# First network of a two-network kernel: weight loads placed around a block's transfers, one semaphore per piece, and an earlier table read

## The reference, cut to what matters

```
# first network (a mixture of experts), N=3072, D=384, E=8, F=1024
expert_idx = argmax(normalised x @ normalised emb.T / tau)
for e in range(E):
    mask = expert_idx == e
    h = np.maximum(x[mask] @ w1[e], 0.0)
    out[mask] = gate_w[mask, None] * (h @ w2[e])
# second network, d_ff = 2048
h = x @ w_in
g = np.maximum(0.01 * h, h)
return g @ w_out
```

## Time and profile before

| What | Value |
|---|---|
| Median of 3 runs | 834.14 us (833.15 to 834.78) |
| Profiled execution, its own time | 836.12 us |
| Its span in the trace | 834.1 us |
| PE busy | 808.0 us, 97% of the span |
| DVE, ACT, POOL busy | 452.2, 345.8, 210.7 us |
| Mean granted TensorE clock | 0.992 |
| First network, about | 132.6 to 427.9 us of the span |

### The profile page before, as it was taken

The page is one execution under the profiler, slowest core; times in us unless marked ns, Lnnn a source line. Parts: engine busy times, 40 slices in busy tenths (PEclk is TensorE's granted clock), DMA queues, the critical chain, the costliest instruction groups (busy, mean ns, idle before and its releaser), DMA issues.

```text
span 834.1 us, 17016 instructions
## 1 busy us (share of the span) xinstructions
PE 808.0 (97%) x5259; PEld 721.7 (87%) x5260; DVE 452.2 (54%) x705; ACT 345.8 (41%) x643; POOL 210.7 (25%) x278
## 2 busy tenths in 40 slices
PE   7999999989989999899999999999999999999998
PEld 6888887978879989788889998998998998998997
DVE  7999986776467474574465433433533433443332
ACT  3555564555346354353254333323323333333223
POOL 5666623233234242332124003003003001000100
PEclk9999999999999999899999999999999999999999
DMA  9997663676787767887733201201101001000001
GB/s 224 261 265 238 202 218 131 219 265 202 285 289 245 245 224 232 283 235 257 222 91 41 39 1 39 39 1 38 28 10 38 0 0 38 1 1 8 30 1 39
DMA packets 64128, 108.97 MB, mean 131 GB/s; under 512 B 24199, under 2 KB 45747, under 8 KB 64080
## 3 DMA queue, kind: packets, MB, share of 16 engines
q1 hardware_dynamic: 54896, 93.47, 37.0%
q0 software_dynamic: 5888, 14.85, 5.6%
q10 hardware_dynamic: 3296, 0.06, 0.2%
HBM read 78.89 MB, written 30.85 MB: 132 GB/s over the span
## 4 chain that ended last, share of the span: by engine, by line
PE 64%; DMA 21%; SPq 6%; issue 4%; DVE 4%; POOL 1%; ACT 1%; DVEq 0%; POOLq 0%; ACTq 0%
PE bank L1747 24%; PE bank L1699 24%; DMA hidden_rows<-hs 18%; PE bank L1494 3%; PE bank L1534 3%; PE bank L1511 2%; PE bank L1672 2%; SPq L448 2%; PE bank L1652 2%; SPq L410 2%; PE bank L1500 1%; PE bank L1542 1%; DMA hds<-hidden_rows 1%; SPq L555 1%; PE bank L1554 1%
## 5 line engine op out<-in xcount | busy, mean ns | idle before, releaser
L1699 PE MATMUL bank<-yT,wts 128*128 128x512 f32 x864 | 217.1, 395 | 0.0
L1747 PE MATMUL bank<-wts,gs 128*128 128x384 f32 x1152 | 215.3, 335 | 0.4 <-ACT os L1010 0.2
L1747 PEld LDWEIGHTS bank<-wts,gs 128*128 128x128 f32 x1152 | 202.1, 188 | 10.7 <-issue 1.6
L1699 PEld LDWEIGHTS bank<-yT,wts 128*128 128x128 f32 x864 | 160.8, 188 | 30.6
L1289 DVE TENSOR_TENSOR g<-bank,small 128x512 f32<-128x512 f32 x96 | 66.4, 692 | 173.6 <-ACT small L919 173.5
L1652 PE MATMUL bank<-wts,gxT 128*128 (+1 forms) x549 | 137.8, 405 | 4.7 <-issue 4.7
L919 ACT ACTIVATE small<-bank 128x512 f32<-128x512 f32 x96 | 57.6, 599 | 184.7 <-PE bank L1699 184.2
L1652 PEld LDWEIGHTS bank<-wts,gxT 128*128 128x128 f32 x549 | 103.8, 194 | 28.1 <-issue 7.0
L1461 DVE TENSOR_TENSOR gs<-g,gs 128x512 fp32r<-128x512 f32 x96 | 66.6, 693 | 66.3 <-ACT gs L1021 66.3
L770 POOL DMA_INDIRECT out<-os,tokens x20 | 19.7, 986 | 285.5 <-ACT os L1010 280.9
L1021 ACT ACTIVATE gs<-g 128x512 fp32r<-128x512 f32 x96 | 60.7, 632 | 74.0 <-DVE g L1289 72.9
(11 more groups left out here) (179 smaller groups left out, 764.7 us busy)
## 6 DMA issues: line engine op xcount, KB each, us to landing
raw<-weights SPq DMA_DIRECT2D x60, 512.0 KB, 6.3
hidden_rows<-hs SPq DMA_DIRECT2D x29, 512.0 KB, 4.9
hds<-hidden_rows SPq DMA_DIRECT2D x29, 512.0 KB, 4.1
qkas<-qka SPq DMA_DIRECT2D x20, 675.5 KB, 5.9
vs<-v SPq DMA_DIRECT2D x24, 192.0 KB, 4.7
x_rows<-xs SPq DMA_DIRECT2D x24, 192.0 KB, 3.7
yl<-y_rows SPq DMA_DIRECT2D x20, 192.0 KB, 4.7
qkas<-qka SPq DMA_DIRECT2D x4, 227.5 KB, 6.8
```

Source lines behind the costliest of these rows:

```text
L1699: m = pe.matmul(gps[f % 2][:, :], wts[:, 0, w_part, n:n + P], yT[:, 1 - u, y_part, k], start=(k == 0 and (w_part, y_part) == (0, 0)), stop ...
L1747: m = pe.matmul(ops[tt], gs[:, f % 4, g_part, tt * P:(tt + 1) * P], wts[:, 1, w_part, f * D:(f + 1) * D], start=(f == 0 and (g_part, w_par ...
```

## The change

Weight loads: `load_half` becomes three calls of `load_piece`, and every piece has a semaphore of its own (`raw_in[0..5]`, count 16 per expert instead of 48 per half). A piece's load waits only for the rounding of the same piece of the expert before (`w_lo[half] >= n*3 - 2 + j`).

SP order: `load_next(m)` with all its loads becomes `load_next(m, j)` with one piece j of each half. It is called three times for a window: in front of the store (j=0), between the issue of the store and the wait for it (j=1), and behind the issue of the read (j=2). Each call reads the table again. The W2 load that was unconditional at window 5 is now at window 4. The four `load_quarter(1, j)` move from behind windows 27 to 30 to behind the loop.

Rounding order: on ACT and DVE the first two pieces of W1 are rounded ahead of `h_round`/`h_rest` of window w+1; the third W1 piece and W2 follow as before. In step 1 `h_round(2)`/`h_rest(2)` and `copy_ys` now come before the rounding of W2 instead of after.

PE: the expert numbers (table reads) of the step's hidden blocks and of window w are read at the start of the step, ahead of the waits for turned rows and weights.

```
         def split_hi(act, n, par, pieces):
             for j in pieces:
-                if j % 3 == 0:
-                    act.wait_ge(raw_in[j // 3], n * 48 + 48)
+                act.wait_ge(raw_in[j], n * 16 + 16)
...
+        def load_piece(eng, half, n, j):
+            eng.wait_ge(w_lo[half], n * 3 - 2 + j)
+            src = weights[n, half] if isinstance(n, int) else weights[ds(n, 1), half].rearrange("a p n -> (a p) n")
+            at = half * 3 + j
+            eng.dma_start(raw[:, at * PC:(at + 1) * PC], src[:, j * PC:(j + 1) * PC]).then_inc(raw_in[at], 16)
...
-            def load_next(m):
+            def load_next(m, j):
...
                 code = table(sp, m - 4)
                 last_first, fourth_first = sp.snap(code & (8 * E)), sp.snap(code & E)
                 with sp.If(last_first > 0):
-                    load_half(sp, 0, sp.snap((table(sp, m - 1) & (E - 1)) + 2))
+                    load_piece(sp, 0, sp.snap((table(sp, m - 1) & (E - 1)) + 2), j)
                 if isinstance(m, int) and m == FIRST + 2:
-                    return
-                if isinstance(m, int) and m == FIRST + 3:
-                    load_half(sp, 1, sp.snap((code & (E - 1)) + 2))
-                else:
+                    load_piece(sp, 1, sp.snap((table(sp, 1) & (E - 1)) + 2), j)
+                elif not (isinstance(m, int) and m == FIRST + 3):
                     with sp.If(fourth_first > 0):
-                        load_half(sp, 1, sp.snap((code & (E - 1)) + 2))
+                        load_piece(sp, 1, sp.snap((code & (E - 1)) + 2), j)
...
+            def move(w, u):
+                load_next(w, 0)
                 sp.wait_ge(h_turned, w * 2 - 2 * FIRST + 2)
...
                 sp.dma_start(h_rows[u], hs[:, u]).then_inc(h_stored[u], 16)
+                load_next(w, 1)
                 sp.wait_ge(h_stored[u], passed(w, u))
...
                 sp.dma_start(hds[:, u].rearrange("p (i n) -> p i n", i=QUADS), h_quarters[u]).then_inc(h_moved[u], 16)
+                load_next(w, 2)
...
-                elif w >= WINDOWS - QUADS:
-                    load_quarter(1, w - WINDOWS + QUADS)
+            wait_rows(1)
+            for j in range(QUADS):
+                load_quarter(1, j)
...
# ACT, and DVE alike with split_lo and h_rest
+                if ahead(w, 3) and not (isinstance(w, int) and w < CLOSE):
+                    with act.If(first3 > 0):
+                        first_weights(w + 3, act.snap(e + first1 // (2 * E) + first2 // (4 * E) + 2), W1_PIECES[:2])
+                if ahead(w, 1) and not (isinstance(w, int) and w == 0):
                     for half in range(2):
                         h_round(w + 1, 1 - u, half)
...
-                        first_weights(w + 3, act.snap(e + first1 // (2 * E) + first2 // (4 * E) + 2))
+                        first_weights(w + 3, act.snap(e + first1 // (2 * E) + first2 // (4 * E) + 2), W1_PIECES[2:])
...
# PE
             def step(w, u):
+                blocks = [(block, of(w, u, block), expert_of(block)) for block in hidden_blocks(w)]
+                e = expert_of(w)
```

More of the change, by code:

```diff
@@ L255, in build @@
         state_ready = sem("state_ready")
-        raw_in = [sem("raw_in0"), sem("raw_in1")]
+        raw_in = [sem(f"raw_in{j}") for j in range(PIECES)]
         w_hi = [sem("w1_hi"), sem("w2_hi")]
@@ L441, in split_lo @@
                                   ALU.subtract).then_inc(w_lo[j // 3], 1)
+        def load_piece(eng, half, n, j):
[3 more added lines that the diff above has]
+            eng.dma_start(raw[:, at * PC:(at + 1) * PC], src[:, j * PC:(j + 1) * PC]).then_inc(raw_in[at], 16)
         def load_half(eng, half, n):
-            eng.wait_ge(w_lo[half], n * 3)
-            src = weights[n, half] if isinstance(n, int) else weights[ds(n, 1), half].rearrange("a p n -> (a p) n")
             for j in range(3):
-                eng.dma_start(raw[:, (half * 3 + j) * PC:(half * 3 + j + 1) * PC],
-                              src[:, j * PC:(j + 1) * PC]).then_inc(raw_in[half], 16)
+                load_piece(eng, half, n, j)
         W1_PIECES, W2_PIECES = range(0, 3), range(3, 6)
@@ L513, in load_first @@
                 sp.dma_start(raw[:, c * PC:(c + 1) * PC],
-                             weights[0, half, :, part * PC:(part + 1) * PC]).then_inc(raw_in[half], 16)
+                             weights[0, half, :, part * PC:(part + 1) * PC]).then_inc(raw_in[c], 16)
             def step(c, b):
@@ L543, in _ @@
                 load_half(sp, half, 1)
-            def move_h(w, u):
+            def load_next(m, j):
+                if isinstance(m, int) and m == FIRST:
+                    with sp.If(sp.snap(table(sp, 0) & (2 * E)) > 0):
+                        load_piece(sp, 0, 3, j)
+                    return
+                if isinstance(m, int) and m == FIRST + 1:
+                    with sp.If(sp.snap(table(sp, 0) & (4 * E)) > 0):
+                        load_piece(sp, 0, sp.snap((table(sp, m - 1) & (E - 1)) + 2), j)
+                    with sp.If(sp.snap(table(sp, 0) & (2 * E)) > 0):
+                        load_piece(sp, 1, 2, j)
+                    return
+                code = table(sp, m - 4)
+                last_first, fourth_first = sp.snap(code & (8 * E)), sp.snap(code & E)
+                with sp.If(last_first > 0):
+                    load_piece(sp, 0, sp.snap((table(sp, m - 1) & (E - 1)) + 2), j)
+                if isinstance(m, int) and m == FIRST + 2:
+                    load_piece(sp, 1, sp.snap((table(sp, 1) & (E - 1)) + 2), j)
+                elif not (isinstance(m, int) and m == FIRST + 3):
+                    with sp.If(fourth_first > 0):
+                        load_piece(sp, 1, sp.snap((code & (E - 1)) + 2), j)
+            def move(w, u):
+                load_next(w, 0)
                 sp.wait_ge(h_turned, w * 2 - 2 * FIRST + 2)
@@ L613, in _ @@
                 move(w, w % 2)
-                if w in (20, WINDOWS - QUADS):
-                    wait_rows(w // (WINDOWS - QUADS))
+                if w == 20:
+                    wait_rows(0)
                 if w < 20 + QUADS:
                     load_quarter(0, w - 20)
-                elif w >= WINDOWS - QUADS:
-                    load_quarter(1, w - WINDOWS + QUADS)
+            wait_rows(1)
+            for j in range(QUADS):
+                load_quarter(1, j)
             for j in range(2):
@@ L894, in h_round, with first_weights @@
                 act.activation(by_square(ht_of(w, u)[:, 0, cols]), moved(u, half), ACT.Copy).then_inc(ht_hi, 1)
-            def first_weights(s, e):
+            def first_weights(s, e, pieces=W1_PIECES):
                 wait_from(act, h_ready, s * 2)
-                split_hi(act, e, next_set(act, e), W1_PIECES)
+                split_hi(act, e, next_set(act, e), pieces)
             def second_weights(w, e):
@@ L960, in step @@
                     scale_small(0)
-                if ahead(w, 1) and not (isinstance(w, int) and w < FIRST):
+                if ahead(w, 3) and not (isinstance(w, int) and w < CLOSE):
+                    with act.If(first3 > 0):
+                        first_weights(w + 3, act.snap(e + first1 // (2 * E) + first2 // (4 * E) + 2), W1_PIECES[:2])
+                if ahead(w, 1) and not (isinstance(w, int) and w == 0):
                     for half in range(2):
@@ L982, in step @@
                         second_weights(w, act.snap(e + 1))
-                if isinstance(w, int) and w == 1:
-                    for half in range(2):
-                        h_round(w + 1, 1 - u, half)
                 if not ahead(w, 1):
@@ L1422, in step @@
                     leaky(0)
-                if ahead(w, 1) and not (isinstance(w, int) and w < FIRST):
+                if ahead(w, 3) and not (isinstance(w, int) and w < CLOSE):
+                    with dve.If(first3 > 0):
+                        e2 = dve.snap(e + first1 // (2 * E) + first2 // (4 * E) + 2)
+                        split_lo(dve, e2, next_set(dve, e2), W1_PIECES[:2])
+                if ahead(w, 1) and not (isinstance(w, int) and w == 0):
                     for half in range(2):
                         h_rest(w + 1, 1 - u, half)
-                if not (isinstance(w, int) and w < FIRST):
+                if not (isinstance(w, int) and w == 0):
                     copy_ys(w, u)
@@ L1441, in step @@
                         split_lo(dve, e1, next_set(dve, e1), W2_PIECES)
-                if isinstance(w, int) and w < FIRST:
+                if isinstance(w, int) and w == 0:
                     copy_ys(w, u)
-                if isinstance(w, int) and w == 1:
-                    for half in range(2):
-                        h_rest(w + 1, 1 - u, half)
                 if isinstance(w, int) and w == WINDOWS - 2:
@@ L1701, in inner, with expert_of, block_hidden @@
                 m.then_inc(g_ready, 1)
-            def block_hidden(s, u, between=None):
-                e = pe.snap(table(pe, s) & (E - 1))
+            def expert_of(w):
```

(8 more changed lines are left out.)

22 lines of the change are left out of this document (2 added, 20 removed).

## The result

The changed kernel takes 828.25 us (median of 6 runs, 827.35 to 830.51) against 834.77 us for the kernel before: ratio 0.9921, 95% interval 0.9897 to 0.9945. It is faster by 6.5 us. The profiled execution took 827.88 us, its span is 826.1 us. The forecast was 825.

The account below looks back on a forecast made before the run. The prediction took SP's serial loop of stores, waits, reads and loads to pace the first network; its terms, 30.3 - 3.0 - 2.0 - 33.5 - 6 + 4 + 1.3 = -8.9 us, gave 825 us, 8-in-10 range 817 to 838.

Parts of the forecast that it names:

- The bound: First network: SP's serial loop of store, wait, read, table and loads sets the pace, 9.4 us a window against PE's 8.6.
- A: SP's loop: the added table-reading call behind the read is on the path in all 25 windows, +30.3 us.
- B: SP's load issues: one in three now lies under the store, W1's second table read is paid twice; -3.0 us.
- C: Quarter loads: three that stood in front of the stores of windows 28, 29, 30 leave the loop; -2.0 us.
- D: SP's stores with fewer loads in front, six becoming two and three becoming one, window 5 included: -33.5 us.
- E: Next store behind a read: later issue queues less, -6 us; third pieces standing in between cost +4 us.
- the third rival: SP's queue: same bytes, what one store gains the next loses, terms cancel, 834 us; chance 0.11.
- F: Start, step 1: W2 rounded behind h_round(2) makes window 5's data later, +1.3 us.
- window 5's term: Window 5's store: its W2 load moves to window 4, so six loads in front become one; -5.5 us.
- edits costed at nothing: Rounding order, PE's earlier table reads and finer load_piece waits: no gain unless SP gets as fast as PE.
- the slower case: Queue between a block's read and the next store: third pieces take the gain back, mostly 836 to 846 us; chance 0.20.
- PE's floor: First network: SP's loop falls below PE's pace, SP waits for DVE, time 816 to 819 us; chance 0.13.

Follow-up runs that it names:

- front_lean: Changed kernel with all loads in front of the store again, in one pass, all other edits kept: 829.83 us, ratio 0.9933 to the kernel before.
- all_in_front: kept_regs with all three pieces of each half in front of the store, in one pass: ratio 0.9982 to the kernel before.
- extra_pass: Changed kernel plus a fourth table read and two branches, never loading, behind each window's read: 838.24 us against 830.41 for after2.
- round_only: Kernel before with only the new rounding order on ACT and DVE: 0.45% faster (0.25 to 0.65).
- pe_only: Kernel before with only PE's table reads moved to the start of the step: 0.32% faster (0.04 to 0.59).
- read_under_store: Changed kernel with one table-reading pass, between store and wait; pieces 0 and 1 there, piece 2 behind the read from kept registers: 817.95 us.
- kept_regs: Changed kernel, but the call behind the read uses registers kept from the call under the store, without table read: ratio 0.9798 to the kernel before.
- sp_only: Kernel before with only SP's part: piece semaphores, load_next in three passes, W2 load at window 4, quarter loads behind the loop: 1.04% faster (0.66 to 1.42).
- after2: The changed kernel unaltered, measured once more beside its variants: 830.41 us, ratio 0.9918 to the kernel before.

## Why the prediction was right, and where its terms were not

**The bound.** Right: SP's loop paced the kernel before; SP's part alone makes it faster, with PE's gaps left in. In the changed kernel steps taken from the loop and put under the store's wait still make it faster, and steps added make it slower.

**A, the passes.** The steps grew by 27.2 us (73.4 to 100.6), predicted 30.3 - 3.0 - 2.0 = 25.3 for A, B and C together.

**D and E, the stores.** Predicted -33.5 - 6 + 4 = -35.5, measured -33.7. By kind, predicted and measured in the changed kernel: six loads a window 6.8 and 6.8 (6.6, 6.2, 7.4, 7.0), three 5.8 and 5.8, window 5 5.8 and 6.1. The stores behind third pieces rose by 4.3 us in sum, predicted 4; the others without loads fell by 4.6, predicted 6. The size of every term was near.

Their causes were less so. I treated A as paid in full and E as a small correction. The experiments show both tied together: a part of the time between read and store comes back as a shorter store, 87% of it from front_lean to all_in_front and 42% in extra_pass. Placement and passes together sum to nothing that can be told (front_lean against changed), and the third rival's mechanism, in which what one transfer gains the next loses, is near that. Its time of 834 was wrong, since the rest of the change, which by C, F and half of window 5's term was to bring some 3 us, is worth 0.67% (front_lean against before, 0.41 to 0.93), 5.5 us.

**C and the edits costed at nothing.** Together these are the mis-sized terms, but which of them isn't settled. The quarter loads were to bring 2.0 us and measure 0 to 10. The rounding order and PE's reads, which I gave nothing unless SP gets as fast as PE, brought 0.45% and 0.32% alone, and nothing measurable on top of SP's part. That PE catches up and waits for SP was argued from the last window; the chain after shows that PE itself leads up to 290 us.

**F, the start.** Predicted 1.3 us, measured 0.2 (window 5's store at 181.78 instead of 181.61). The rounding order alone moved it by just 1.3 (182.87 in round_only), and PE's earlier reads, which the prediction left out here, by 1.3 the other way (180.28 in pe_only).

**The sum.** The loop was predicted 10.2 shorter and is 6.4 shorter (A to E); from the last store to the last contraction it is 9.3 us instead of 11.0, which the prediction held fixed. The total fits: -8.9 predicted, -8.0 in the span, -6.5 in the medians. It fits partly because the omitted gain of the side edits and the overrated gain of the placement stand against each other.

**The signs.** I said that SP would wait for stores for some 115 to 120 us; it was 74.5. I took the shorter stores off the 149.8 and forgot the call that A itself puts under the store: of the 128.2 us of stores SP now spends over 50 in its own work. Steps without loads of 3.0 us, the last contraction near 419 and the vanished "issue" gaps came as said. One sign of being wrong came too: three of the eight stores behind third pieces took over 6 us (windows 9, 23 and 26), while their mean is 5.2.

**The rivals.** The third pieces cost 4.3 us, or 0.3 a piece, not 1.2: the slower case didn't come, but extra_pass shows that 0.6 us more a window brings its time about by another way. PE's floor was reached in full by read_under_store. Its mark, SP waiting for `hs` and the chain in PE, was there in kept_regs and already in sp_only, with three table reads a window; so the argument that these reads keep SP too slow for it was wrong, and the whole change came near it up to 290 us only.

Of the cost of a single transfer, the shortest stores of these profiles take 2.6 us, with no load in front. The Trainium skill, in "DMA: Bandwidth & Descriptors" (Anatomy of one DMA — SWDGE (gpsimd) path, its two cost components; the prediction names another section), gives about 2.0 us fixed plus the bytes over 436 GB/s, which for 512 KB is an estimate of 3.2 us. It was fitted there on GpSimd's path, and these stores are SP's. The measured 2.6 us is less, and decides. With the Trainium skill's figure the stores would have had less left to give back, 1.2 instead of 1.8 us a window.

## What to carry to other kernels

Where one sequencer waits, transfers and waits again, first put its own work (table reads, branches, issues) between the issue and the wait, once, and keep the results in registers; splitting loads over three places pays only if the places don't each read and branch anew. Count a step between two transfers of one queue together with the queue time of the transfer behind it, since much of the one turns into the other. And test side edits apart from the main one: here the kernel with the side edits alone (front_lean) has a gain that can't be told from that of the whole, and the placement of the loads, the main edit, just paid for its own passes.

## What the runs showed of the hardware that was not expected

A store's time from issue to release fell, on average, with its distance from the read in front of it: over the fifteen windows without loads 4.4 us at a mean distance of 1.9 (before) and 3.8 at the same distance (front_lean), 3.0 at 3.2 (all_in_front). The two values at 1.9 show that distance isn't the only cause. Below 2.6 no store of 512 KB went in any of the 14 profiles.

One pass is not like another: a table read and two branches not taken took SP 0.8 to 1.5 us, 1.1 on average, as the third call of `load_next` (seven windows, before against changed), and some 0.6 us in extra_pass (3.43 us from read to store at window 7 against 2.83 in after2). Why is open.
